# Two gated networks on one TensorE: the low tail weights of gate and value as two 64-row matmuls

## The chip, the cores and the metric

One NeuronCore of one Trainium2 chip. The metric is the device time of one execution in microseconds (us); three runs of the kernel before gave 1295.91, 1297.44 and 1297.57, median 1297.44.

## What is computed

```python
# x: (2, 4096, 192); 8 heads of 24 channels; softmaxed 7-tap causal filter per head
out = np.einsum('hk,bskhg->bshg', w, x_unf)         # token mixing
# first network: 8192 tokens, 192 -> 1536 -> 192
g = x @ w_gate
val = x @ w_val
x = (g * sigmoid(g) * val) @ w_out
# second network: 192 -> 2048 -> 192
h = x @ w_in
y = elu(h) @ w_out2
```

Everything is float32. The change touches the two products `x @ w_gate` and `x @ w_val` alone.

## The kernel before, in words

The 8192 tokens are worked on in 16 chunks of 512, channels on the partitions. TensorE computes with the rounded type fp32r, so each factor is split into a high part (the rounded value) and a low part (what rounding left), and a product is built from several matmuls: high by high, low weights by high data, high weights by low data. The 192 channels are cut into a main part of 128 and a tail of 64. For the tail the 128 rows of the array are filled by keeping the 64 channels twice: `in_b_tail` (in chunk 0 `in_a_tail`) holds the high part of the data in rows 0 to 63 and its low part in rows 64 to 127, and the weights `tail_hi` and `tail_lo` hold the same 64 rows twice. One matmul with `tail_hi` so gives high by high plus high by low, and one with `tail_lo` gives low by high plus low by low. The tile named plain `tail_hi` (not that of a weight) holds the high part of the tail data in both halves; until now only VectorE read it, to make `in_b_tail`.

The hidden layer is worked in blocks of 128 units (f in the first network, 12 of them; k in the second, 16). For a block of the first network TensorE issues ten matmuls of 512 columns: for the gate `main_hi` by high, `main_lo` by high, `main_hi` by low, `tail_hi`, `tail_lo` (`project_up`, which calls `project_main` and `project_tail`, lines 771 to 790), and the same five for the value. The last of each five raises `gate_ready` or `val_ready`. On `gate_ready` ScalarE makes SiLU (line 467), on that and `val_ready` VectorE multiplies (line 634, which raises `mul_done`), ScalarE rounds the product to `hid_hi` (line 480), GpSimd makes `hid_lo` (line 384), and three blocks later TensorE multiplies them with the output weights (`down1`, five matmuls). In the second network a block is five matmuls up and eight shorter ones down (`down2`).

Every engine runs a program of its own, in the order written, and they meet at semaphores. On TensorE it is `mix_phase(0)`, `mix_phase(1)`, a loop of `elu_phase(n)` and `mix_phase(n+1)` for n from 1 to 14, then `elu_phase(15)` and `elu_phase(16)`. A mix phase is the first network of a chunk (with the filter of the next chunk on VectorE), an elu phase the second network of the chunk before. The first block of an elu phase begins with `down1` of block 9 and then waits until the products of all 12 blocks are made, since its bank of PSUM is the value bank of block 11. Gate and value alternate between two banks each. All matmuls pass through the helper `mm`, so all have line 769.

```python
pe.wait_ge(in2_hi, 2 * n)
pe.wait_ge(in2_lo, 2 * n)
if k >= 3:
    pe.wait_ge(elu_done, N2 * (n - 1) + k - 2)
elif last:
    pe.wait_ge(elu_done, N2 * (n - 1) - 2 + k)
elif k == 0:
    pe.wait_ge(mul_done, N1 * (n + 1))
```

Chunk 0 has a piece of its own for its first block, and its phase also takes in the weights as they are loaded; the change leaves chunk 0 as it is.

Of the kernel before, what the change touches and what calls it, by code (L numbers as in the profile page):

```python
# [28 lines left out]
P = 128  # L29


def mix_ffn_ffn(nc, x, weight, w_gate, w_val, w_out1, w_in2, w_out2, out):
# [10 lines left out]
    TAIL = D - P  # L43
# [23 lines left out]
    with ctx:  # L67
        def sb(name, shape, dt=F32):
            return ctx.enter_context(nc.sbuf_tensor(name, shape, dt))

        def sem(name):
            return ctx.enter_context(nc.semaphore(name))


        def split_weight(name, cols):
            return {part: sb(f"{name}_{part}", [P, cols], F32R)
                    for part in ("main_hi", "main_lo", "tail_hi", "tail_lo")}

        gate_w = split_weight("gate_w", F1)
        val_w = split_weight("val_w", F1)  # L80
# [31 lines left out]
        tail_hi = sb("tail_hi", [P, 2, T], F32R)  # L112
# [21 lines left out]
        def input1(c):  # L134
            return in_a if is_int(c, 0) else in_b
# [4 lines left out]
        def is_int(n, value):  # L140
            return isinstance(n, int) and n == value

        def gate_bank(f):
            return up[3] if f % 2 == 0 else up[2]

        def val_bank(f):
            return up[1] if f % 2 == 0 else up[0]
# [24 lines left out]
        gate_ready = sem("gate_ready")  # L172
        val_ready = sem("val_ready")
# [101 lines left out]
        def wait_weights(eng, upto):  # L275

            eng.wait_ge(piece_hi, upto)
            for who, made in (("dve", piece_lo_dve), ("pool", piece_lo_pool)):
                if lo_count(upto, who):
                    eng.wait_ge(made, lo_count(upto, who))  # L280
# [486 lines left out]
        def _(pe):  # L767
            def mm(dst, lhsT, rhs, start, stop):
                return nc.tensor.matmul(dst, lhsT, rhs, start=start, stop=stop, skip_group_check=True)  # L769

            def project_main(bank, w, data, f, lo_ready=None):

                c = slice(f * P, (f + 1) * P)
                mm(bank[:, :], w["main_hi"][:, c], data["hi"][:, :], True, False)
                mm(bank[:, :], w["main_lo"][:, c], data["hi"][:, :], False, False)
                if lo_ready:
                    pe.wait_ge(in1_lo, lo_ready)
                mm(bank[:, :], w["main_hi"][:, c], data["lo"][:, :], False, False)

            def project_tail(bank, w, data, f):  # L780

                c = slice(f * P, (f + 1) * P)
                mm(bank[:, :], w["tail_hi"][:, c], data["tail"][:, :], False, False)
                return mm(bank[:, :], w["tail_lo"][:, c], data["tail"][:, :], False, True)

            def project_up(bank, w, data, f):
                project_main(bank, w, data, f)
                return project_tail(bank, w, data, f)

            def down1(n, f):  # L790


                a, z = f == 0, f == N1 - 1
                hi, lo = hid_hi[:, f % RING, :], hid_lo[:, f % RING, :]
                main_hi, tails = out1_w[:, f, 0:P], out1_w[:, f, P:2 * P]
                main_lo = out1_w[:, f, 2 * P:3 * P]
                if a and is_int(n, 1):
                    pe.wait_ge(y_main_done, 1)
                    pe.wait_ge(halves_done, 1)
                elif a and not is_int(n, 0):  # L800
                    pe.wait_ge(result_done, SUB * (n - 2) + 2)
                if f == 1 and not (is_int(n, 0) or is_int(n, 1)):
                    pe.wait_ge(result_done, SUB * (n - 1))
                pe.wait_ge(hi1_done, N1 * n + f + 1)
                mm(ACC_MAIN[:, :], main_hi, hi, a, False)
                mm(ACC_MAIN[:, :], main_lo, hi, False, False)
                mm(ACC_TAIL[:, :], tails, hi, a, False)
                pe.wait_ge(lo1_done, N1 * n + f + 1)
                mm(ACC_MAIN[:, :], main_hi, lo, False, z)
                mm(ACC_TAIL[:, :], tails, lo, False, z).then_inc(down1_done, 1)  # L810

            def down2(m, k, bank_free=None):


                a, z = k == 0, k == N2 - 1
                pe.wait_ge(hi2_done, N2 * m + k + 1)
                for s in OUT_ORDER if is_int(m, CHUNKS - 1) else range(SUB):
                    if a:
                        bank_free(s)
                    mm(down[s][:, 0:2 * D], hid_hi[:, k % RING, s * P:(s + 1) * P], out2_w[:, k, :], a, False)  # L820
                if is_int(m, CHUNKS - 1) and z:
                    pe.wait_ge(last_lo_done, 1)
                else:
                    pe.wait_ge(lo2_done, N2 * m + k + 1)
                for s in OUT_ORDER:
                    last = mm(down[s][:, 0:D], hid_lo[:, k % RING, s * P:(s + 1) * P], out2_w[:, k, 0:D],
                              False, z)
                    if z:
                        last.then_inc(y_ready, 1)
                if not z:  # L830
                    last.then_inc(down2_done, 1)

            def mix_phase(n):
                chunk0, chunk1 = is_int(n, 0), is_int(n, 1)
                for f in range(N1):
                    if f < LAG:
                        if chunk1:
                            down1(0, N1 - LAG + f)
                        elif not chunk0:
                            down2(n - 2, N2 - LAG + f)  # L840
                    else:
                        if chunk0 and (f - LAG) % OT == 0:
                            wait_weights(pe, (UP_A + 1, OUT_B, PIECES1)[(f - LAG) // OT])
                        down1(n, f - LAG)
                    if chunk0:
                        for g, made in enumerate((UP_A, UP_B, UP_C)):
                            if f * P == GROUPS[g][0]:
                                wait_weights(pe, made)
                    if f == 0 and chunk0:

                        pe.wait_ge(in1_hi, 1)
                        project_main(gate_bank(0), gate_w, in_a, 0, lo_ready=1)
                        project_main(val_bank(0), val_w, in_a, 0)
                        pe.wait_ge(in1_hi, 2)
                        pe.wait_ge(in1_lo, 2)
                        project_tail(gate_bank(0), gate_w, in_a, 0).then_inc(gate_ready, 1)
                        project_tail(val_bank(0), val_w, in_a, 0).then_inc(val_ready, 1)
                        continue
                    if f == 0:
                        pe.wait_ge(in1_hi, 2 * n + 2)  # L860
                        pe.wait_ge(in1_lo, 2 * n + 2)

                    if f >= 2 or chunk1:
                        pe.wait_ge(silu_done, N1 * n + f - 1)
                    elif f == 1 and not chunk0:
                        pe.wait_ge(elu_done, N2 * (n - 2) + N2 - 1)
                    project_up(gate_bank(f), gate_w, input1(n), f).then_inc(gate_ready, 1)
                    if f >= 2 or chunk1:
                        pe.wait_ge(mul_done, N1 * n + f - 1)
                    elif not chunk0:  # L870
                        pe.wait_ge(elu_done, N2 * (n - 2) + N2 - 2 + 2 * f)
                    project_up(val_bank(f), val_w, input1(n), f).then_inc(val_ready, 1)

            def elu_phase(n):
                last = is_int(n, CHUNKS)
# [49 lines left out]
            for k in range(PAIRS):  # L925
                pe.wait_ge(diag_done, k + 1)
                last = mm(MIX0[:, :], diag[:, k, :], paired[:, 2 * k:2 * k + T], k == 0, k == PAIRS - 1)
            last.then_inc(mix0_ready, 1)
            mix_phase(0)
            mix_phase(1)  # L930
            with pe.Fori(1, CHUNKS - 1) as n:
                elu_phase(n)
                mix_phase(n + 1)
# [22 lines left out]
```

## Time and profile before

| | |
|---|---|
| median of three runs | 1297.44 us (1295.91 to 1297.57) |
| profiled execution, span from first to last instruction | 1295.2 us |
| mean granted TensorE clock | 0.998 |
| TensorE matmul busy | 1281.8 us (99%), 6240 matmuls |
| weight loads busy (beside matmuls) | 1084.1 us (84%) |
| VectorE, ScalarE, GpSimd busy | 798.4, 665.3, 656.5 us (62%, 51%, 51%) |
| DMA, mean | 22 GB/s |

The profiled execution lists no time of its own beside its span; the span is 2.2 us under the median of the runs. A matmul's record is longer than the distance to the next one, since matmuls are pipelined: the distance between two starts is what it costs, the record includes the way of the last column to PSUM. Weight loads (PEld) run beside matmuls and have records of their own. A record's start is when the instruction was issued; if its weights are not there yet the record is longer.

### The profile page before, as it was taken

To read this page: it belongs to the slowest core of one execution; us is meant where nothing else is said; L and a number is where in the kernel's file an instruction comes from. 1 tells how busy PE (TensorE), PEld (TensorE's weight loads), DVE (VectorE), ACT (ScalarE), POOL (GpSimd) and SP (SyncE) were. 2 spreads that over 40 slices of the span, in tenths; PEclk is the share of its full clock that TensorE was granted. 3 is DMA by queue.
4 is the path that set the end of the run, shared out by engine and by line. 5 is a ranking of instruction groups with operands and counts; after the bars stand their busy time and mean duration, and the time that the engine had idled before them with its cause. 6 is when DMAs were issued, how large, how long until landed. Compare 5 with 4: busy or idle time off the path is not lost.

```text
span 1295.2 us, 19686 instructions
## 1 busy us (share of the span) xinstructions
PE 1281.8 (99%) x6240; PEld 1084.1 (84%) x6240; DVE 798.4 (62%) x1196; ACT 665.3 (51%) x1104; POOL 656.5 (51%) x477
## 2 busy tenths in 40 slices
PE   7999999999999999999999999999999999999998
PEld 5888888888888888888888888888888888888887
DVE  7667566664665756557565665656666466574675
ACT  5455545455453544545455454554545546355454
POOL 5574445454454544545455454454545545454454
PEclk9999999999999999999999999999999999999999
DMA  8221001010010100101000010100101001010000
GB/s 190 56 75 25 13 9 16 12 24 12 8 21 7 24 12 8 28 0 24 12 14 22 3 21 12 24 12 8 16 12 24 12 8 16 12 24 12 9 13 13
DMA packets 93858, 28.15 MB, mean 22 GB/s; under 512 B 77456, under 2 KB 90256, under 8 KB 93840
## 3 DMA queue, kind: packets, MB, share of 16 engines
q1 hardware_dynamic: 93840, 27.93, 9.6%
q8 instruction: 9, 0.15, 0.1%
q14 instruction: 9, 0.07, 0.0%
HBM read 17.43 MB, written 6.29 MB: 18 GB/s over the span
## 4 chain that ended last, share of the span: by engine, by line
PE 96%; DVE 2%; issue 1%; ACT 0%; POOL 0%; POOLq 0%; DVEq 0%; ACTq 0%
PE up L769 57%; PE down L769 39%; DVE mixed L742 1%; DVE mixed L576 0%; ACT act L498 0%; DVE hidden L634 0%; DVE act L673 0%; DVE hidden L692 0%; DVE out_w L296 0%; ACT out_w L289 0%; DVE in_a_lo L582 0%; POOLq L67 0%; DVE hidden L735 0%; POOL hid_lo L384 0%; POOL head_of L368 0%
## 5 line engine op out<-in xcount | busy, mean ns | idle before, releaser
L384 POOL TENSOR_TENSOR hid_lo<-hidden,hid_hi 128x512 fp32r<-128x512 f32 x447 | 631.0, 1412 | 625.8 <-ACT hid_hi L480 351.0
L634 DVE TENSOR_TENSOR hidden<-act,up 128x512 f32<-128x512 f32 x192 | 131.5, 685 | 275.6 <-ACT act L467 248.5
L519 ACT ACTIVATE hid_hi<-hidden 128x512 fp32r<-128x512 f32 x256 | 162.0, 633 | 209.0 <-DVE hidden L692 209.0
L480 ACT ACTIVATE hid_hi<-hidden 128x512 fp32r<-128x512 f32 x192 | 121.5, 633 | 258.7 <-DVE hidden L634 258.7
L692 DVE SCALAR_TENSOR_TENSOR hidden<-act,up 128x512 f32<-128x512 f32 x256 | 175.9, 687 | 121.8 <-ACT act L498 117.3
L769 PE MATMUL down<-out_w,hid_hi 128*128 128x384 f32 x1024 | 222.9, 339 | 0.4 <-DVE result L619 0.2
L673 DVE TENSOR_SCALAR act<-up 128x512 f32<-128x512 f32 x256 | 176.6, 690 | 63.8 <-PE up L769 58.5
L769 PEld LDWEIGHTS down<-out_w,hid_hi 128*128 128x128 f32 x1024 | 186.7, 188 | 24.2 <-issue 0.6
L498 ACT ACTIVATE act<-act 128x512 f32<-128x512 f32 x256 | 161.3, 630 | 45.7 <-DVE act L673 39.8
L467 ACT ACTIVATE act<-up 128x512 f32<-128x512 f32 x192 | 114.7, 597 | 103.0 <-PE up L769 102.7
L769 PE MATMUL down<-hid_hi,out_w 128*128 128x512 f32 x576 | 166.1, 396 | 0.0
L769 PEld LDWEIGHTS down<-out_w,hid_lo 128*128 128x128 f32 x1024 | 149.2, 189 | 3.8 <-POOL hid_lo L384 3.5
L769 PE MATMUL down<-out_w,hid_lo 128*128 128x192 f32 x1024 | 151.4, 270 | 0.1
L576 DVE SCALAR_TENSOR_TENSOR mixed<-x_t,taps,mixed 128x512 f32<-128x512 f32 x192 | 140.3, 771 | 0.0
L769 PEld LDWEIGHTS down<-hid_hi,out_w 128*128 128x128 f32 x576 | 108.4, 188 | 26.6
L769 PE MATMUL down<-hid_lo,out_w 128*128 128x512 f32 x384 | 121.1, 396 | 0.0
L769 PE MATMUL up<-in_a_hi,in_w_main_hi 128*128 128x512 f32 x240 | 98.7, 411 | 1.6 <-DVE hidden L634 1.6
L769 PE MATMUL up<-in_a_tail,in_w_tail_hi 128*128 128x512 f32 x240 | 95.6, 398 | 0.0
L769 PE MATMUL up<-in_a_lo,in_w_main_hi 128*128 128x512 f32 x240 | 94.7, 395 | 0.0
L769 PE MATMUL up<-in_a_tail,in_w_tail_lo 128*128 128x512 f32 x240 | 94.6, 394 | 0.0
L769 PE MATMUL up<-in_a_hi,in_w_main_lo 128*128 128x512 f32 x240 | 94.5, 394 | 0.0
L769 PEld LDWEIGHTS down<-hid_lo,out_w 128*128 128x128 f32 x384 | 72.3, 188 | 17.6
(141 smaller groups left out, 1772.3 us busy)
## 6 DMA issues: line engine op xcount, KB each, us to landing
x_raw<-x_dram SPq DMA_DIRECT2D x144, 64.0 KB, 2.2
out_dram<-result SPq DMA_DIRECT2D x15, 384.0 KB, 2.6
swapped<-halves SPq DMA_DIRECT2D x32, 128.0 KB, 2.3
stage<-w_out_dram SPq DMA_DIRECT2D x7, 384.0 KB, 3.4
stage<-w_in_dram SPq DMA_DIRECT2D x4, 256.0 KB, 2.9
stage<-w_in_dram SPq DMA_DIRECT2D x8, 128.0 KB, 2.9
stage<-w_gate_dram SPq DMA_DIRECT2D x4, 192.0 KB, 4.0
stage<-w_val_dram SPq DMA_DIRECT2D x4, 192.0 KB, 4.2
```

Source lines behind the costliest of these rows:

```text
L384: return pool.tensor_tensor(hid_lo[:, slot, :], hidden[:, s, :], hid_hi[:, slot, :].bitcast(F32), ALU.subtract)
L467: nc.scalar.activation(act[:, f % 2, :], gate_bank(f)[:, :], ACT.Silu)\
L480: nc.scalar.activation(hid_hi[:, f % RING, :], hidden[:, f % 2, :], ACT.Copy)\
L498: nc.scalar.activation(act[:, k % 2, :], act[:, k % 2, :], ACT.Exp).then_inc(exp_done, 1)
L519: nc.scalar.activation(hid_hi[:, k % RING, :], hidden[:, k % 2, :], ACT.Copy)\
L576: v.scalar_tensor_tensor(mixed[:, part, :], src, tap, mixed[:, part, :], ALU.mult, ALU.add).then_inc(mix_step, 1)
L634: v.tensor_tensor(hidden[:, f % 2, :], act[:, f % 2, :], val_bank(f)[:, :], ALU.mult)\
L673: v.tensor_scalar(act[:, k % 2, :], elu_bank(n, k)[:, :], 0.0, None, ALU.min)\
L692: v.scalar_tensor_tensor(hidden[:, k % 2, :], act[:, k % 2, :], -1.0, elu_bank(n, k)[:, :], ALU.add, ALU.max).then_inc(elu_done, 1)
L742: v.scalar_tensor_tensor(mixed[:, 0, :], src, tap0, mixed[:, 0, :], ALU.mult, ALU.add)\
L769: return nc.tensor.matmul(dst, lhsT, rhs, start=start, stop=stop, skip_group_check=True)
```

## The change

In chunks 1 to 15 the last matmul of the gate and the last of the value are taken out of their places. The value's four others are issued, and then the two low tail products together: the gate's on rows 0 to 63 of the array, the value's on rows 64 to 127, each with 64 rows of weights and of high tail data (`tail_hi[..., 0, :]`). The built program gives both a tile of 64 by 128 of the array, at row 0 and at row 64; all other matmuls of 128 rows have the full tile. The product of low weights by low data is left out. The number of matmuls stays. `gate_ready` is now raised after the value's matmuls too.

```diff
+            def project_most(bank, w, data, f):
+
+                c = slice(f * P, (f + 1) * P)
+                project_main(bank, w, data, f)
+                mm(bank[:, :], w["tail_hi"][:, c], data["tail"][:, :], False, False)
+
+            def project_lo_pair(f):
+
+                c = slice(f * P, (f + 1) * P)
+                top, low = slice(0, TAIL), slice(TAIL, P)
+                mm(gate_bank(f)[:, :], gate_w["tail_lo"][top, c], tail_hi[top, 0, :], False, True)\
+                    .then_inc(gate_ready, 1)
+                mm(val_bank(f)[:, :], val_w["tail_lo"][low, c], tail_hi[low, 0, :], False, True)\
+                    .then_inc(val_ready, 1)
...
-                    project_up(gate_bank(f), gate_w, input1(n), f).then_inc(gate_ready, 1)
+                    if chunk0:
+                        project_up(gate_bank(f), gate_w, input1(n), f).then_inc(gate_ready, 1)
+                    else:
+                        project_most(gate_bank(f), gate_w, input1(n), f)
                     if f >= 2 or chunk1:
                         pe.wait_ge(mul_done, N1 * n + f - 1)
                     elif not chunk0:
                         pe.wait_ge(elu_done, N2 * (n - 2) + N2 - 2 + 2 * f)
-                    project_up(val_bank(f), val_w, input1(n), f).then_inc(val_ready, 1)
+                    if chunk0:
+                        project_up(val_bank(f), val_w, input1(n), f).then_inc(val_ready, 1)
+                    else:
+                        project_most(val_bank(f), val_w, input1(n), f)
+                        project_lo_pair(f)
```

How this moves TensorE's instructions, at an ordinary block of chunk 1. Before:

```order
L769 MATMUL up<-in_b_tail,gate_w_tail_hi 128x512
L769 MATMUL up<-in_b_tail,gate_w_tail_lo 128x512
L769 MATMUL up<-in_b_hi,val_w_main_hi 128x512 [waits mul_done]
L769 MATMUL up<-in_b_hi,val_w_main_lo 128x512
L769 MATMUL up<-in_b_lo,val_w_main_hi 128x512
L769 MATMUL up<-in_b_tail,val_w_tail_hi 128x512
L769 MATMUL up<-in_b_tail,val_w_tail_lo 128x512
L769 MATMUL down<-hid_hi,out_w 128x512 [waits hi1_done]
```

And now, where the shape shown is that of the output:

```order
L769 MATMUL up<-in_b_tail,gate_w_tail_hi 128x512
L769 MATMUL up<-in_b_hi,val_w_main_hi 128x512 [waits mul_done]
L769 MATMUL up<-in_b_hi,val_w_main_lo 128x512
L769 MATMUL up<-in_b_lo,val_w_main_hi 128x512
L769 MATMUL up<-in_b_tail,val_w_tail_hi 128x512
L769 MATMUL up<-tail_hi,gate_w_tail_lo 128x512
L769 MATMUL up<-tail_hi,val_w_tail_lo 128x512
L769 MATMUL down<-hid_hi,out_w 128x512 [waits hi1_done]
```

The gate's last matmul, which completes its bank, moved behind four matmuls of the value; the two with `tail_lo` now stand side by side between full-array ones.

The second place is where the mix phase of chunk 1 ends on TensorE and the first elu phase begins. Now:

```order
L769 MATMUL up<-in_b_tail,val_w_tail_hi 128x512
L769 MATMUL up<-tail_hi,gate_w_tail_lo 128x512
L769 MATMUL up<-tail_hi,val_w_tail_lo 128x512
L953 UNCONDITIONAL_BRANCH
...
L769 MATMUL down<-hid_hi,out_w 128x512 [waits hi1_done]
L769 MATMUL down<-hid_hi,out_w 128x512 x2
L769 MATMUL down<-hid_lo,out_w 128x512 [waits lo1_done]
L769 MATMUL down<-hid_lo,out_w 128x512
...
L769 MATMUL up<-in_a_hi,in_w_main_hi 128x512 [waits mul_done]
```

Between the two low tail matmuls of block 11 and the wait for its product stand five matmuls, as before; but then the gate's bank was complete five matmuls earlier still.

## Rows read from the trace of the kernel before

**Rows 1.** The page: busy time of each engine, granted clock in 40 slices.
```profile
PE 1281.8 (99%) x6240; PEld 1084.1 (84%) x6240; DVE 798.4 (62%) x1196; ACT 665.3 (51%) x1104; POOL 656.5 (51%) x477
...
PE   7999999999999999999999999999999999999998
...
PEclk9999999999999999999999999999999999999999
```
**Rows 2.** The page: the chain that ended last, by engine.
```profile
PE 96%; DVE 2%; issue 1%; ACT 0%; POOL 0%; POOLq 0%; DVEq 0%; ACTq 0%
```
**Rows 3.** Groups of TensorE instructions, the replaced ones: count | busy us, mean ns | idle.
```profile
L769 PE MATMUL up<-in_b_tail,gate_w_tail_lo 128*128 128x512 f32 x180 | 71.5, 397 | 0.0
...
L769 PE MATMUL up<-in_b_tail,val_w_tail_lo 128*128 128x512 f32 x180 | 71.2, 396 | 0.0
```
**Rows 4.** Timeline of TensorE, one block of a mix phase: start us, duration us.
```profile
626.44 0.39 PE L769 MATMUL up<-in_b_hi,gate_w_main_hi 128*128 128x512 f32 x1
...
628.31 0.39 PE L769 MATMUL up<-in_b_tail,val_w_tail_hi 128*128 128x512 f32 x1
628.54 0.40 PE L769 MATMUL up<-in_b_tail,val_w_tail_lo 128*128 128x512 f32 x1
628.78 0.86 PE L769 MATMUL down<-hid_hi,out_w 128*128 128x512 f32 x3
...
629.95 0.39 PE L769 MATMUL up<-in_b_hi,gate_w_main_hi 128*128 128x512 f32 x1
```
**Rows 5.** Timeline of weight loads and matmuls at the start, across a change of rows.
```profile
5.59 0.54 PEld L769 LDWEIGHTS down<-taps_head,head_of 8*128 8x128 f32 x2
5.66 0.57 PE L769 MATMUL down<-taps_head,head_of 8*128 8x7 f32 x2
...
6.15 0.29 PEld L769 LDWEIGHTS up<-fold 128*128 128x128 f32 x1
6.15 0.58 PE L769 MATMUL up<-fold 128*128 128x128 f32 x1
```
**Rows 6.** All matmuls with `fold`: duration min/median/max ns.
```profile
L769 PE MATMUL up<-fold x20: 324/421/582, 4.1 to 9.5; 128*128 128x128 f32 x20
```
**Rows 7.** Timeline of TensorE and its weight loads, where the first elu phase waited.
```profile
102.10 0.19 PEld L769 LDWEIGHTS up<-in_a_hi,in_w_main_hi 128*128 128x128 f32 x1 [2.03 <-DVE hidden L634]
102.10 0.50 PE L769 MATMUL up<-in_a_hi,in_w_main_hi 128*128 128x512 f32 x1 [1.59 <-DVE hidden L634]
102.21 0.19 PEld L769 LDWEIGHTS up<-in_a_hi,in_w_main_lo 128*128 128x128 f32 x1
102.43 0.39 PE L769 MATMUL up<-in_a_hi,in_w_main_lo 128*128 128x512 f32 x1
```
**Rows 8.** Timeline of all engines, the end of a mix phase.
```profile
655.49 0.40 PE L769 MATMUL up<-in_b_tail,gate_w_tail_lo 128*128 128x512 f32 x1
...
655.92 0.60 ACT L467 ACTIVATE act<-up 128x512 f32<-128x512 f32 x1 [0.93 <-PE up L769]
...
656.66 0.40 PE L769 MATMUL up<-in_b_tail,val_w_tail_lo 128*128 128x512 f32 x1
...
657.15 0.69 DVE L634 TENSOR_TENSOR hidden<-act,up 128x512 f32<-128x512 f32 x1 [2.75 <-ACT act L467]
...
657.89 0.19 PEld L769 LDWEIGHTS up<-in_a_hi,in_w_main_hi 128*128 128x128 f32 x1
658.06 0.39 PE L769 MATMUL up<-in_a_hi,in_w_main_hi 128*128 128x512 f32 x1
```
**Rows 9.** Timelines of VectorE and weight loads, the third block of a mix phase.
```profile
623.72 1.15 DVE L619 TENSOR_TENSOR result<-result,down 128x192 f32<-128x192 f32 x4 [0.99 <-ACT result L455]
...
625.03 0.66 PEld L769 LDWEIGHTS down<-hid_hi,out_w 128*128 128x128 f32 x3
```

## The prediction

> **What bounds the kernel now.** I read the page's busy times and granted clock first: TensorE is busy 99% of the span, in every slice but the first, at the full clock of 2.4 GHz (0.998 granted) [rows 1]. The chain that ended last says the same: 96% of it is TensorE [rows 2]. So whatever lengthens or shortens the stream of matmuls moves the time one for one, and other engines count only where TensorE comes to wait for them. Then the groups of matmuls: the two that the change replaces are 180 of the gate and 180 of the value (15 chunks by 12 blocks), with no idle time ahead of them [rows 3]. Their mean of 396 ns is a record, not a cost. The cost is read from the timeline: one block has 15 matmuls of 512 columns and takes 629.95 - 626.44 = 3.51 us, so 0.234 us each [rows 4]. A record of 0.395 us thus has 0.234 us of columns and 0.16 us of way to PSUM.
>
> **The change, part by part.**
>
> *Two full matmuls become two of 64 rows.* If both stream at once, on their two halves of the array, a pair takes 0.234 us where two took 0.469: 180 x 0.234 = 42.1 us less. That is the gross gain, and the whole of it is on the path.
>
> *Full array to halves and back.* The array is cut differently for the pair, so each block gets two changes of cut. The trace before has just one in a stream without a wait: at the start two small matmuls of 8 rows are followed by full-array ones with `fold` [rows 5]. Normally a weight load runs beneath the matmul before it, as the load at 102.21 does, whose matmul starts at 102.43 [rows 7]. Across the change it did not: load and matmul both start at 6.15. The last 8-row record ends at 5.66 + 0.57 = 6.23, its columns were through at 6.23 - 0.16 = 6.07. So the load was held for 0.08 us after the columns were through, and the matmul then waited for its weights: its record is 0.58 us where the median with `fold` is 0.42 [rows 6], 0.16 more. For the fp32r matmuls of this change the price of a load that nothing hides is better read where the first elu phase had waited: 0.50 us against the 0.39 of the next [rows 7], 0.11. I take 0.08 + 0.11 = 0.19 us for a change of cut, and 0.08 + 0.16 = 0.24 as the upper end. The lower end is nothing: it is one event, of fp32 matmuls and an 8-row cut, and it need not hold here. I take the row since it is the only one in which the cut changes. Two changes per block: 0.38 us (0 to 0.48).
>
> The Trainium skill, "TensorEngine Tiling (Array Packing)", Tiling Modes, speaks against this change too: changing the tiling mode, not just the tile, drains TensorE. It has no duration for the drain; the row agrees with it.
>
> *How far the two halves overlap.* The value's half needs its own weights. Behind a change of cut no load was made early, so two loads come one after the other. The nearest distance of two loads with nothing between is 102.21 - 102.10 = 0.11 us [rows 7]. I take 0.11 us by which the value's half starts and ends later; ends are 0 (loads of different rows at once) and 0.234 (one half after the other, no overlap).
>
> By the Trainium skill, "TensorE: Matmul & The Clock Gate", Part 3, matmuls on different row groups start about 4 ns apart; no row of before shows it. By that the skew would be near nothing and the sum 1329 us in place of 1347, the low end of my own case worked out below.
>
> *Per block:* 0.38 + 0.11 - 0.234 = +0.256 us. With 180 blocks: **+46.1 us**. With skew 0: +0.146, 26.3 us. With 0.24 per change and the skew: +0.356, 64.1 us.
>
> *Low by low left out* saves nothing by itself: a matmul of 64 rows streams as many columns.
>
> *The gate's bank is complete later.* Inside a mix phase this has slack: the same bank is asked for two blocks on, and all else on the chain (SiLU, product, rounding, low part) has until three blocks on; the other engines are busy 51 to 62% [rows 1]. There are two tight places. The first is the end of each mix phase. Before, the gate's SiLU started at 655.92, long before the value was ready; the value's last record ended at 656.66 + 0.40 = 657.06, the product started 0.09 later and ended at 657.84, and the elu phase's first weight load started at 657.89, its matmul at 658.06 [rows 8]. Since a load needs 0.11, the matmul could have started at 658.00: 0.06 us of slack. Now SiLU starts only when the pair is through: 0.03 (655.92 after 655.89) + 0.60 + about 0.05 until VectorE sees it puts the product 0.68 us after the pair's end in place of 0.09, so 0.59 later. Were nothing else changed, TensorE would wait 0.59 - 0.06 = 0.53 us. But in my case the gate's half is through 0.11 earlier than the value's, and the five matmuls between start 0.19 later because of the change of cut: 0.53 - 0.11 - 0.19 = 0.23 us, in each of the 15 phases: **+3.5 us**. Queued behind that wait on TensorE is the whole elu phase; nothing catches it up.
>
> The second is the third block, where `down1` needs banks that VectorE reads in the result additions; two of these four must be done, at 623.72 + 1.15/2 = 624.30, and the load stands at 625.03 [rows 9]. ScalarE's copies ahead of them come 0.59 later: 624.89. TensorE comes later too in my case, so this costs nothing. What hides it is 0.14 us of slack; without the changes of cut, `down1` would come 0.234 earlier and wait about 0.1 us, 14 times, 1.4 us.
>
> No DMA, no load and no instruction of the other engines changes, and the granted clock stays at its upper level, since a gap of 2.03 us [rows 7] left no slice with a lower clock [rows 1].
>
> **Sum:** 46.1 + 3.5 = +49.6 us on the median of 1297.4: **1347 us**. The durations are those of the execution with a span of 1295.2 us, 2.2 us under that median; the same distance is kept.
>
> **The rivals.**
>
> *Faster: the change of cut costs nothing.* Loads for 64 rows are made early like any other, because each block has room for two loads (0.11 each) beneath one matmul (0.234). For it: the only evidence against it is one event [rows 5] with another type of matmul. Then -42.1, plus 15 x 0.53 = 8.0 for the ends of the phases and 1.4 for the third blocks: -32.7, 1265 us. If the value's load does wait for the gate's half to start (skew 0.11): 180 x -0.124 = -22.3, plus 15 x 0.42 = 6.3: -16.0, 1281 us. This decides at 0.12 us per change of cut: two of them use up 0.234 us, and above that the pair is slower than the two it replaces.
>
> *The halves don't overlap, and the cut is paid:* 180 x 0.38 = 68.4, plus 15 x (0.53 - 0.23 - 0.19) = 1.6: +70, 1367 us. Against it: two halves of different rows and different banks have nothing to share.
>
> *The change does not do what it says:* the halves are run like full matmuls, one after the other, at no price for the cut. Then nothing is gained per block, and the late gate costs 15 x (0.53 - 0.23) = 4.5 us: 1302 us. A cheap change of cut (0.1 us) with a skew lands beside it, between 1295 and 1310.
>
> **How the numbers follow.** My case, cut paid and halves beside each other, 0.55: from 26.3 + 15 x (0.53 - 0.19) = 31.4, 1329 us, to 64.1 + 15 x (0.53 - 0.11 - 0.24) = 66.8, 1364 us. Faster rival 0.28, in two halves at 1265 and 1281. No overlap 0.07. Near no change 0.10, of which 0.04 within 0.2% (2.6 us, about what a measurement of this kernel can tell from no change) and 0.06 slower. So faster 0.28, same 0.04, slower 0.55 + 0.07 + 0.06 = 0.68. The range takes in the faster rival and goes up to 1362: it leaves out the rival without overlap and the top of my own case, some 0.13 in all. It is wide because the cases of both signs need it; the likeliest one's own range is 1329 to 1364.
>
> **What would show each step.** In the timeline of a block: matmul with `tail_hi` of the value, then a load of 64 rows that starts no sooner than 0.3 us after it (right: cut paid) or beneath it (wrong). The two halves' starts 0.11 us or less apart, by records of 64 rows. The load of the next `down1` 0.3 us after the halves' start, not beside them. A block of 3.77 us in place of 3.51; 3.28 would be the faster rival. At the phase ends, TensorE idle ahead of `in_a_hi,in_w_main_hi`, released by VectorE line 634, some 0.1 to 0.5 us, 15 times. The prediction is wrong if the loads of the halves lie beneath full matmuls, or if the halves start 0.234 us apart.

## The result, and the profile after

| | before | after |
|---|---|---|
| median of three runs | 1297.44 us | 1330.01 us (1327.41 to 1330.26) |
| ratio | | 1.0246, 95% interval 1.0227 to 1.0264 |
| span of the profiled execution | 1295.2 us | 1328.5 us |
| mean granted TensorE clock | 0.998 | 0.997 |

The change makes the kernel slower by 32.6 us, 2.5%; the forecast was 49.6 us slower, 1347 us, in a range that goes from the faster rival up to 1362 us.

The page of the kernel after, busy times and chain by engine. Against [rows 1] and [rows 2] matmul records cover more time and weight loads less (78% for 84%); the chain is TensorE's as before. The clock is at its upper level in all slices but the first, which is looked at below:

```profile
PE 1314.7 (99%) x6240; PEld 1036.9 (78%) x6240; DVE 797.7 (60%) x1196; ACT 667.7 (50%) x1104; POOL 653.8 (49%) x477
...
PEclk8999999999999999999999999999999999999999
...
PE 96%; DVE 2%; issue 1%; ACT 0%; POOL 0%; POOLq 0%; DVEq 0%; ACTq 0%
```

The replaced matmuls of the kernel after, in groups (count | busy us, mean ns | idle before), to be read against [rows 3]: the records went from 397 to 493 ns.

```profile
L769 PE MATMUL up<-tail_hi,gate_w_tail_lo 64*128 64x512 f32 x180 | 88.8, 493 | 0.0
L769 PE MATMUL up<-tail_hi,val_w_tail_lo 64*128 64x512 f32 x180 | 88.7, 493 | 0.0
```

The timeline of TensorE in a block of the kernel after (start us, duration us), which answers to [rows 4]:

```profile
642.99 0.39 PE L769 MATMUL up<-in_b_hi,gate_w_main_hi 128*128 128x512 f32 x1
...
644.63 0.40 PE L769 MATMUL up<-in_b_tail,val_w_tail_hi 128*128 128x512 f32 x1
644.95 0.49 PE L769 MATMUL up<-tail_hi,gate_w_tail_lo 64*128 64x512 f32 x1
644.96 0.49 PE L769 MATMUL up<-tail_hi,val_w_tail_lo 64*128 64x512 f32 x1
645.38 0.97 PE L769 MATMUL down<-hid_hi,out_w 128*128 128x512 f32 x3
...
646.65 0.40 PE L769 MATMUL up<-in_b_hi,gate_w_main_hi 128*128 128x512 f32 x1
```

And its weight loads:

```profile
644.39 0.19 PEld L769 LDWEIGHTS up<-in_b_tail,val_w_tail_hi 128*128 128x128 f32 x1
644.95 0.18 PEld L769 LDWEIGHTS up<-tail_hi,gate_w_tail_lo 64*128 64x128 f32 x1 [0.36 <-issue]
644.95 0.18 PEld L769 LDWEIGHTS up<-tail_hi,val_w_tail_lo 64*128 64x128 f32 x1
645.38 0.53 PEld L769 LDWEIGHTS down<-hid_hi,out_w 128*128 128x128 f32 x3 [0.24 <-issue]
```

A block now takes 646.65 - 642.99 = 3.66 us for 3.51. Into the pair: the value's matmul with `tail_hi` starts at 644.63, its columns are through 0.234 later, at 644.86, the loads of the pair start at 644.95 (0.09 held), and the pair's records are 0.49 for 0.39 (0.10 of waiting for weights). Out of it: the halves' columns are through at 644.95 + 0.10 + 0.23 = 645.28, the next load starts at 645.38 (0.10 held), and the first of the three matmuls of `down1` has its weights 0.11 later (three take 0.97 us for 0.86). Together 0.40; from the block, 3.66 + 0.234 - 3.51 = 0.38 (the sums below use 0.388). Both halves start and end together: their loads start within 0.01 us. By the records the pair's load starts 0.08 us ahead of the end of the matmul before it (644.63 + 0.40 = 645.03), so it isn't held until that matmul has ended; ends of matmuls are modelled in these profiles, so this is less sure than the starts.

The end of a mix phase in the kernel after, all engines, against [rows 8]:

```profile
674.29 0.49 PE L769 MATMUL up<-tail_hi,val_w_tail_lo 64*128 64x512 f32 x1
...
674.82 0.60 ACT L467 ACTIVATE act<-up 128x512 f32<-128x512 f32 x1 [1.68 <-PE up L769]
...
675.45 0.69 DVE L634 TENSOR_TENSOR hidden<-act,up 128x512 f32<-128x512 f32 x1 [2.90 <-ACT act L467]
...
676.19 0.19 PEld L769 LDWEIGHTS up<-in_a_hi,in_w_main_hi 128*128 128x128 f32 x1 [0.47 <-DVE hidden L634]
676.19 0.50 PE L769 MATMUL up<-in_a_hi,in_w_main_hi 128*128 128x512 f32 x1
```

SiLU starts 0.04 us behind the pair (674.82 against 674.78), the product waits for it, ends at 676.14, and the elu phase's first load follows; the matmul waits for its weights besides. From the last pair of matmuls of `down1` (0.63 us, of which 0.47 is cost, from 675.52) TensorE would have gone on at 675.99; it had its weights at 676.19 + 0.10. The loss is 0.3 us per phase.

The first and last start of the value's low tail matmul, by tile, in the kernel before and the kernel after:

```profile
L769 PE MATMUL up<-in_b_tail,val_w_tail_lo x180: 390/397/400, 60.3 to 1212.1; 128*128 128x512 f32 x180
```

```profile
L769 PE MATMUL up<-tail_hi,val_w_tail_lo x180: 491/492/502, 62.1 to 1244.7; 64*128 64x512 f32 x180
```

Between first and last the time grew from 1151.8 to 1182.6 us: 30.8. That is 179 blocks at 0.154 us (0.388 in and out, less 0.234), 27.6, and some 0.3 us at 14 phase ends less what the end of chunk 1, which waits for VectorE anyway, takes back. Of the 33.3 us between the spans 1.8 lie ahead of the first pair, in code that the change doesn't touch. There the clock was at its lower level for longer. Busy times and granted clock (the third figure from the right) from 16 to 24 us, in the kernel before and the kernel after; from there to the first pair the clock is 1.00 in both:

```profile
16.00:24.00 8.00, 7.37 (x25) 5.48 (x26) 7.94 (x12) 5.41 (x9) 3.27 (x3) 0.79 1.14 219
```

```profile
16.00:24.00 8.00, 6.78 (x16) 5.08 (x17) 7.92 (x11) 5.15 (x9) 3.28 (x3) 0.57 1.00 205
```

In both a part of these 8 us was granted at 1.2 GHz, behind a stretch in which TensorE had waited 3 us for the first chunk's data, and the rest at 2.4 GHz. A mean of 0.79 over 8 us costs 0.21 x 8 = 1.7 us of work, one of 0.57 costs 3.4, so the difference is 1.7 of the 1.8 us. The kernel before also has runs between 1295.9 and 1299.0, so a few microseconds in a comparison of two runs can be the clock's; times between two starts later in the trace, such as the 3.66 us, don't have this uncertainty.

### The profile page after: what moved, and what is told of

Its sections match the earlier page's. It is cut to its first block, busy times and chain, and to the rows that moved or that the text cites. A ratio compares the mean times of both kernels' runs of the same rounds, so it can differ in the third digit from the quotient of the medians.

```text
span 1328.5 us, 19686 instructions
## 1 busy us (share of the span) xinstructions
PE 1314.7 (99%) x6240; PEld 1036.9 (78%) x6240; DVE 797.7 (60%) x1196; ACT 667.7 (50%) x1104; POOL 653.8 (49%) x477
## 4 chain that ended last, share of the span: by engine, by line
PE 96%; DVE 2%; issue 1%; ACT 0%; POOL 0%; POOLq 0%; DVEq 0%; ACTq 0%
PE up L769 55%; PE down L769 41%; DVE mixed L742 1%; DVE mixed L576 0%; DVE hidden L634 0%; ACT act L498 0%; DVE act L673 0%; DVE hidden L692 0%; DVE out_w L296 0%; ACT out_w L289 0%; DVE in_a_lo L582 0%; POOLq L67 0%; DVE hidden L735 0%; POOL hid_lo L384 0%; POOL head_of L368 0%
## 5 line engine op out<-in xcount | busy, mean ns | idle before, releaser
L769 PE MATMUL down<-out_w,hid_hi 128*128 128x384 f32 x1024 | 225.8, 342 | 0.3 <-DVE result L619 0.2
L769 PE MATMUL down<-hid_hi,out_w 128*128 128x512 f32 x576 | 182.1, 424 | 0.0
L769 PEld LDWEIGHTS down<-hid_hi,out_w 128*128 128x128 f32 x576 | 96.5, 188 | 48.8 <-issue 32.7
L769 PE MATMUL up<-tail_hi,gate_w_tail_lo 64*128 64x512 f32 x180 | 88.8, 493 | 0.0
```

## The experiments

The theory: every change between the full array and halves of it costs about 0.19 us, half of it a hold of the next load until the columns before are through, half a load that nothing hides; the halves themselves overlap fully; the late gate is a small rest. The rivals: a large part of the loss is the late gate; the price belongs to the two halves beside each other; halves are slow in themselves. The kernel before was run beside each set, with a median of 1297.6 us each time.

### The order of the change without the halves

```diff
-                mm(gate_bank(f)[:, :], gate_w["tail_lo"][top, c], tail_hi[top, 0, :], False, True)\
+                mm(gate_bank(f)[:, :], gate_w["tail_lo"][:, c], in_b["tail"][:, :], False, True)\
                     .then_inc(gate_ready, 1)
-                mm(val_bank(f)[:, :], val_w["tail_lo"][low, c], tail_hi[low, 0, :], False, True)\
+                mm(val_bank(f)[:, :], val_w["tail_lo"][:, c], in_b["tail"][:, :], False, True)\
```

> The order of the changed kernel, but both low tail matmuls on the full array with 128 rows of weights and data, as before the change. Theory 1 (each change of the array's cut costs about 0.19 us, and the late gate costs little): without the cuts 180 x 0.388 us go, two full matmuls cost 0.234 us more per block than the pair; what is left over the kernel before is the late gate alone: 15 phase ends of 0.3 to 0.5 us, +4.5 to +8 us, 1302 to 1306 us. Theory 2 (a good part of the 32.6 us is the late gate, the wait for the product at the phase ends and for the result additions): +15 us or more.

Measured 1303.87 us, ratio to before 1.0043 (1.0029 to 1.0056): +5.6 us (6.2 between the medians). The end of a mix phase, all engines:

```profile
661.50 0.40 PE L769 MATMUL up<-in_b_tail,val_w_tail_lo 128*128 128x512 f32 x1
...
661.70 0.60 ACT L467 ACTIVATE act<-up 128x512 f32<-128x512 f32 x1 [1.53 <-PE up L769]
...
663.08 0.19 PEld L769 LDWEIGHTS up<-in_a_hi,in_w_main_hi 128*128 128x128 f32 x1 [0.44 <-DVE hidden L634]
663.08 0.50 PE L769 MATMUL up<-in_a_hi,in_w_main_hi 128*128 128x512 f32 x1
```

At the phase ends the late gate costs this: the elu matmul starts 1.58 us after the value's last in place of 1.40 [rows 8], and waits 0.1 more for its weights, 0.28 us in 15 phases, 4.2. The blocks themselves take 3.51 us as before. The spans of the profiled runs differ by 7.1 us, and most of the other 2.9 can be put down to the clock: its mean was 0.57 over 16 to 24 us (0.79 before) and 0.89 over 100 to 115 us, behind the wait at the end of chunk 1 (1.00 before), worth 1.7 us each. In this run the gate is ready one matmul, 0.234 us, ahead of the value; in the changed kernel it is not, but there the way out of the cut holds the five matmuls between for 0.19 us, so its loss of 0.3 us is nearly the same. So 4 to 5 of the 32.6 us are the gate's, and the rest is the pair's, but for some 1.7 us of clock.

### Halves apart

Each 64-row matmul alone, in the place that its full matmul had before the change:

```diff
-            def project_up(bank, w, data, f):
+            def project_half(bank, w, data, f, rows):
+                c = slice(f * P, (f + 1) * P)
                 project_main(bank, w, data, f)
-                return project_tail(bank, w, data, f)
+                mm(bank[:, :], w["tail_hi"][:, c], data["tail"][:, :], False, False)
+                return mm(bank[:, :], w["tail_lo"][rows, c], tail_hi[rows, 0, :], False, True)
```

> The kernel before, with each low tail matmul left in its old place but with 64 rows (gate on the upper half, value on the lower); low by low is left out. Theory 1 (the price is paid per change of cut): two pairs of changes per block, each 0.388 us, and no overlap: +180 x 0.776 = +140 us, about 1437 us. Theory 2 (the price belongs to the two halves running side by side, for instance that their loads or reads get in each other's way): the single halves cost little, under +20 us.

Measured 1434.66 us (a single run), +137.0 where the theory had +140. Timeline of TensorE in a block:

```profile
639.06 0.40 PE L769 MATMUL up<-in_b_tail,gate_w_tail_hi 128*128 128x512 f32 x1
639.39 0.50 PE L769 MATMUL up<-tail_hi,gate_w_tail_lo 64*128 64x512 f32 x1
639.82 0.50 PE L769 MATMUL up<-in_b_hi,val_w_main_hi 128*128 128x512 f32 x1
640.16 0.40 PE L769 MATMUL up<-in_b_hi,val_w_main_lo 128*128 128x512 f32 x1
```

From 639.06 to 640.16 three matmuls take 1.10 us instead of 3 x 0.234 = 0.70: 0.40 for one way in and out, around a single half with nothing beside it. So the price does not belong to two halves side by side; it is paid where full-array and 64-row matmuls meet. That it is not one of 64-row matmuls as such is shown by the runs with many of them in a row, below.

### Both on the same half

```diff
-                mm(val_bank(f)[:, :], val_w["tail_lo"][low, c], tail_hi[low, 0, :], False, True)\
+                mm(val_bank(f)[:, :], val_w["tail_lo"][top, c], tail_hi[top, 0, :], False, True)\
```

> The changed kernel with both 64-row matmuls on the upper half of the array (the value's weights and data of rows 0 to 63, which hold the same values). Theory 1 (the halves of the changed kernel overlap in full, which gives 0.234 us per block back): the two now stream one after the other with the second load hidden, +180 x 0.234 = +42 us, about 1372 us. Rival (nothing overlapped in the changed kernel either, the records start together but the columns don't): 1330 us as the changed kernel.

Measured 1366.87 us (a single run), 36.9 more than the changed kernel. Groups:

```profile
L769 PE MATMUL up<-tail_hi,gate_w_tail_lo 64*128 64x512 f32 x180 | 89.7, 498 | 0.0
L769 PE MATMUL up<-tail_hi,val_w_tail_lo 64*128 64x512 f32 x180 | 70.7, 393 | 0.0
```

Only the first of the two waits for weights (498 ns); the second's load was hidden (393). 180 x 0.234 = 42.1 us for streaming one after the other, less 15 x 0.234 = 3.5 for the phase ends, where the gate is now ready 0.234 us ahead of the value: 38.6. The last 1.7 us agree with the clock's share: this run had a mean of 0.79 between 16 and 24 us, as the kernel before, and the kernel after 0.57. So in the changed kernel the halves do overlap in full, and the gross gain of 42 us is there; it is the way in and out, 180 x 0.388 = 70 us, that eats it.

### Halves throughout

If only the change of cut is dear, it should be made rarely. In blocks 3 to 11 of chunks 1 to 15 all matmuls that TensorE issues, up and down, are made of an upper and a lower half (the `down1` of the last three blocks, which stand in the elu phase, stay whole); two halves that stand beside each other write different banks, and a semaphore orders the two halves of one bank. Low by low is left out in these blocks; blocks 0 to 2 and the second network are as before the change. The heart of it:

```diff
+                tops = g_top + m_top + t_top + v_top
+                lows = v_low + t_low + g_low + m_low
+                assert len(tops) == len(lows) == 14
...
+                    if slot == 8:
+                        pe.wait_ge(low_done, 3 * before + 2)
...
+                    i = tops[slot]()
...
+                    i = lows[slot]()
```

(g and v are the halves of gate and value, five on one side and four on the other, since a tail half gives high by high, high by low or low by high; m and t are the three main and two tail halves of `down1`.)

> Chunks 1 to 15, blocks 3 to 11 of the first network: every matmul (up and down) is cut into an upper and a lower half of 64 rows, in 14 slots of two halves on different banks instead of 15 full matmuls; low by low left out there. Blocks 0 to 2 are as before the change. The cut changes twice per phase, not twice per block. Theory 1 (only a change of cut holds up loads, in one cut the loads of halves are hidden like any other): -135 x 0.234 + 30 x 0.19 = -26 us, about 1271 us. Theory 2 (64-row matmuls can't have their loads hidden, or four instructions don't fit in a slot of 0.234 us): at least 0.1 us more in each of 135 x 14 slots, over 1450 us; in between, if the slots take 0.25 us, about 1300 us.

Measured 1286.64 us, ratio 0.9915 (0.9900 to 0.9930): faster than before, but some 16 us short of the estimate. Weight loads in a block:

```profile
641.42 0.18 PEld L771 LDWEIGHTS up<-in_b_hi,gate_w_main_hi 64*128 64x128 f32 x1
641.87 0.18 PEld L771 LDWEIGHTS down<-hid_hi,out_w 64*128 64x128 f32 x1 [0.26 <-PE down L771]
641.87 0.18 PEld L771 LDWEIGHTS up<-in_b_hi,gate_w_main_lo 64*128 64x128 f32 x1
```

A load waits for TensorE itself: the upper half of the tail product asks for the end of the lower half on its bank, a slot too early. It and the load beside it start together at 641.87 and are then not hidden. The waits of the whole run:

```profile
PEld down L771 <- PE down L771: 35.9, 135, 0.3
```

135 times, once per block. No other wait in that list comes once per block.

### The same, with that wait a slot later

```diff
-                tops = g_top + m_top + t_top + v_top
+                tops = g_top + m_top + v_top[:1] + t_top + v_top[1:]
...
                     if slot == 8:
-                        pe.wait_ge(low_done, 3 * before + 2)
+                        pe.wait_ge(low_done, 3 * before + 1)
-                    if slot == 10:
-                        pe.wait_ge(low_done, 3 * before + 1)
+                    if slot == 9:
+                        pe.wait_ge(low_done, 3 * before + 2)
...
-                    if slot in (4, 7, 9):
+                    if slot in (4, 7, 10):
```

> As e4_halves_throughout, but the upper halves of the tail product are moved from slots 8 and 9 to 9 and 10 (an upper half of the value takes slot 8), so that the wait for the lower half on the same bank comes a slot later. In e4 that wait held two loads for 0.27 us once per block, 135 times, and its matmuls' records were 0.49 us in place of 0.39. Theory 1 (14 slots of 0.234 us and two changes of cut per phase are all there is): 1286.6 - 135 x 0.10 = 1273 us, near the 1271 first expected. Theory 2 (the rest comes from streams of halves themselves, slots a little longer than 0.234 us): 1283 to 1287 us.

Measured **1274.97 us, ratio 0.9827 (0.9814 to 0.9841)**: 22.6 us less than the kernel before and 55 less than the change. Weight loads from one block to the next:

```profile
640.20 0.18 PEld L771 LDWEIGHTS up<-in_b_lo,gate_w_main_hi 64*128 64x128 f32 x1
640.21 0.18 PEld L771 LDWEIGHTS up<-in_b_lo,val_w_main_hi 64*128 64x128 f32 x1
640.43 0.19 PEld L771 LDWEIGHTS up<-in_b_tail,gate_w_tail_hi 64*128 64x128 f32 x1
640.44 0.18 PEld L771 LDWEIGHTS up<-in_b_tail,val_w_tail_hi 64*128 64x128 f32 x1
...
643.48 0.18 PEld L771 LDWEIGHTS up<-in_b_lo,gate_w_main_hi 64*128 64x128 f32 x1
```

643.48 - 640.20 = 3.28 us for 14 slots, 0.234 each, with two loads and two matmuls in every slot. The full rate holds in halves as in the full array. The estimate was 1273 us, and from chunk 2 on it comes true: a chunk takes 77.63 us (from 182.10 to 259.73, between the starts of two elu phases) for 79.36 (from 181.96 to 261.32) in the kernel before, 1.73 less, where 9 x 0.234 - 0.38 gives 1.73. Chunk 1 gives nothing. At its end TensorE waits for VectorE in the kernel before already [rows 7], the wait only gets longer (3.4 us for 2.0), and behind it the mean granted clock was 0.89 over 100 to 115 us, where the kernel before has 1.00.

### Two blocks in one stretch of halves

The changed kernel, with the four low tail halves of two blocks issued together in blocks 2 to 9; blocks 0, 1, 10 and 11 are as before the change.

```diff
-                    if chunk0:
+                    if chunk0 or f < 2 or f >= 10:
...
                         project_most(val_bank(f), val_w, input1(n), f)
-                        project_lo_pair(f)
+                        if f % 2 == 1:
+                            project_lo_pair(f - 1)
+                            project_lo_pair(f)
```

> The changed kernel, but in blocks 2 to 9 of each phase the 64-row matmuls of two blocks (four halves, four banks) stand in one stretch of the cut; blocks 0, 1, 10 and 11 are as before the change. Theory 1 (in and out of the cut costs 0.388 us whatever stands between, and a pair of halves saves 0.234 us): per two blocks 0.388 - 0.469 = -0.081 us, 4 x 15 times, -4.9 us, 1292 to 1294 us, just faster than before. Theory 2 (each pair of halves carries a price of its own): slower than before, about 1297 + 60 x 0.31 = 1316 us if nothing is shared.

Measured 1305.32 us, ratio 1.0057 (1.0043 to 1.0071): a miss in the time, though the mechanism is there. Timeline of TensorE:

```profile
641.82 0.40 PE L769 MATMUL up<-in_b_tail,val_w_tail_hi 128*128 128x512 f32 x1
642.15 0.50 PE L769 MATMUL up<-tail_hi,gate_w_tail_lo 64*128 64x512 f32 x1
642.15 0.49 PE L769 MATMUL up<-tail_hi,val_w_tail_lo 64*128 64x512 f32 x1
642.49 0.39 PE L769 MATMUL up<-tail_hi,gate_w_tail_lo 64*128 64x512 f32 x1
642.49 0.39 PE L769 MATMUL up<-tail_hi,val_w_tail_lo 64*128 64x512 f32 x1
```

The second pair pays nothing of its own, and two blocks take about 0.07 us less than before. But the elu phases wait longer at their start. Theory 1 was right about the cut and wrong in taking the rest of the kernel as free.

> As e6_two_blocks_per_cut, with blocks 8 and 9 as before the change too, so that only blocks 2 to 7 share cuts in twos. In e6 two blocks together took 6.96 us against 7.03 (the gain expected), but the phase ends waited 0.54 us more and the first of them 3.1 us more. Theory 1 (the loss of e6 is the backlog of products at the phase end, since both products of a group become ready at once two blocks before it): with two more full blocks behind the last group the backlog is gone, 3 x 15 x -0.07 = -3 us, 1294 us. Theory 2 (the loss belongs to the groups, wherever they stand): still slower than before, 1300 us or more.

The edit is `f >= 8` for `f >= 10`. Measured 1305.85 us, ratio 1.0065 (1.0051 to 1.0078): a miss again, and the loss doesn't go away with two more full blocks behind the last group. VectorE's timeline in a mix phase of this kernel:

```profile
650.82 1.78 DVE L582 TENSOR_TENSOR in_a_lo<-y_main,in_a_hi 128x512 fp32r<-128x512 f32 x1
652.53 0.67 DVE L634 TENSOR_TENSOR hidden<-act,up 128x512 f32<-128x512 f32 x1
653.12 1.40 DVE L576 SCALAR_TENSOR_TENSOR mixed<-x_t,taps,mixed 128x512 f32<-128x512 f32 x2
654.45 1.77 DVE L585 SCALAR_TENSOR_TENSOR in_a_tail<-tail_hi,lo_half,y_tail 128x512 fp32r<-128x512 f32 x1
656.15 0.67 DVE L634 TENSOR_TENSOR hidden<-act,up 128x512 f32<-128x512 f32 x1
...
658.67 2.89 DVE L576 SCALAR_TENSOR_TENSOR mixed<-x_t,taps,mixed 128x512 f32<-128x512 f32 x2
661.48 0.67 DVE L634 TENSOR_TENSOR hidden<-act,up 128x512 f32<-128x512 f32 x1
...
663.34 0.69 DVE L634 TENSOR_TENSOR hidden<-act,up 128x512 f32<-128x512 f32 x1 [1.10 <-ACT act L467]
```

In the blocks that also prepare the second network's input, VectorE has 656.15 - 652.53 = 3.62 us of work for a block of 3.51 us: no slack at all. That is so in the kernel before too, where two such products also start 3.62 us apart, and there VectorE catches up in the block behind. Here it doesn't. It works without an idle stretch from 650.82 to 662.24, and two steps of the filter that take 1.40 us elsewhere take 2.89 from 658.67 on. GpSimd's and ScalarE's rows beside them:

```profile
657.57 1.74 POOL L384 TENSOR_TENSOR hid_lo<-hidden,hid_hi 128x512 fp32r<-128x512 f32 x1 [1.89 <-ACT hid_hi L480]
659.49 1.52 POOL L384 TENSOR_TENSOR hid_lo<-hidden,hid_hi 128x512 fp32r<-128x512 f32 x1 [0.18 <-ACT hid_hi L480]
...
662.19 0.63 ACT L480 ACTIVATE hid_hi<-hidden 128x512 fp32r<-128x512 f32 x1 [2.29 <-DVE hidden L634]
662.73 0.58 ACT L467 ACTIVATE act<-up 128x512 f32<-128x512 f32 x1
```

VectorE is behind: the product that starts at 658.07 has had its value bank complete since 655.29 + 0.39 = 655.68. It follows that of 656.15 closely, so GpSimd's two low parts come 0.18 us apart, from 657.57 to 661.01, and the slow filter steps lie beside them. In this trace and in that of the run before, 28 filter steps behind 140 us, two in each of 14 chunks, take 1.2 or 1.8 us in place of 0.74, always in this place, 20.7 us more in all; in all other kernels of this document none does there. The product behind them comes at 661.48, ScalarE, which works in order, can round it only at 662.19, and makes the last SiLU only at 662.73, though its gate was complete at 661.55. So the last product, which the elu phase waits for, is late. VectorE itself stands idle for 1.10 us just ahead of it.

Not all of the loss is there. The spans are 9.0 and 7.8 us longer than that of the kernel before, and 6.0 and 4.6 of these are there by the start of chunk 2 (at 145.85 and 144.44 us, against 139.85): the end of chunk 1 waits 5.1 us for VectorE in place of 2.0, and the mean granted clock behind it is 0.77 and 0.89 over 100 to 115 us, for 1.00. The 14 chunks behind lose 0.2 us each, which is 0.5 at the phase end less what the groups gain. That VectorE, 62% busy on the average, is full just there, and slower beside two low parts in a row, was read from the traces; no run with less work on VectorE or GpSimd was made to show it.

## Why the prediction was right

- **The stream of matmuls sets the time.** Held from chunk 2 on in every run but the last two: the times of a chunk follow from counts of 0.234 us slots, changes of cut and the phase end. In the last two VectorE makes the phase end longer.
- **The gross gain of 42.1 us** is real (37 us come back when the halves share a side, with 3.5 for the phase ends and 1.7 for the clock taken off).
- **The price of a change of cut**, taken from one event at the start of the trace of before [rows 5] and a load that nothing hid [rows 7]: 0.08 + 0.11 = 0.19, twice per block 0.38. Measured 0.38 to 0.40: 0.09 and 0.10 held, 0.10 and 0.11 of waiting for weights. That two rows of other kinds of matmul add up so closely is in part luck; the prediction itself gave 0 to 0.48. The rule of the Trainium skill ("TensorEngine Tiling (Array Packing)", Tiling Modes) that a change of mode drains TensorE agrees with the trace, which shows the next load held for 0.09 to 0.10 us.
- **The skew between the halves, taken as 0.11 us, was the term that was mis-sized.** It is under 0.01 us. The loads of the two halves start together; the distance of 0.11 us in [rows 7] is that of two loads for the same rows, and doesn't hold for different ones. 180 x 0.11 = 19.8 us too much, against a miss of 17.0 in all; the other way went about 1 us at the phase ends and 1.7 us of clock, which no term of the sum had. The estimate given beside the Trainium skill's Part 3 of "TensorE: Matmul & The Clock Gate", 1329 us, was the right one: its rule of nearly equal starts agrees with this trace (644.95 and 644.96).
- **The phase ends**: 0.23 us forecast, about 0.3 measured, since the gate's half is not ahead of the value's (0.53 - 0.19 = 0.34 by the prediction's own terms). 4 to 5 us, not 3.5.
- **The third blocks, nothing:** held. From the start of the third block to that of the fourth, across this `down1`, it is 3.68 us for 3.53 in the kernel before, 0.15 more, as in every other block. The wait that was forecast for the case without a price for the cut was not put to the test.
- **The granted clock** was taken as unchanged. It is from 24 us on; ahead of that its mean was 0.57 for 0.79 in the profiled runs, worth about 1.7 us.

The faster rival (no price for the cut) and the one without overlap are both excluded, by the block of 3.66 us and by the two matmuls on the same half, and so is the case in which the halves are run like full matmuls, whose block would be 3.51 us.

## What to carry to other kernels

Matmuls of 64 rows side by side give all that they promise, a pair for the time of one, but going from full-array matmuls to halves and back costs 0.19 us each way, in the midst of a dense stream, where a full matmul of 512 columns costs 0.234. One pair per stretch of halves loses 0.15 us. Two gain 0.07 us per stretch on TensorE, which here was more than lost again on VectorE. Nine blocks of a phase in halves gain all that was counted, from chunk 2 on (1297.6 to 1275.0 us here). So before a matmul is packed, count the changes of cut, not the matmuls. And where a product is made available later, look at each engine in that stretch rather than at its average: VectorE at 62% had blocks with no slack.

## What the runs showed of the hardware that was not expected

- The loads for two different halves start within 0.01 us of each other, also when neither was made early (644.95 both); loads for the same rows are 0.11 us apart [rows 7].
- In a stretch of halves each slot of 0.234 us takes two loads and two matmuls, and 14 slots take 3.28 us: no loss against the full array.
- A wait of TensorE on its own earlier matmul costs a load that isn't hidden, about 0.1 us, when only one slot lies between; with two no such wait is left in the trace. A chunk with nine such blocks took 78.46 us in the first run and 77.63 in the second, 0.09 per block.
- Steps of the filter on VectorE take 1.2 and 1.8 us in place of 0.74 where two low parts on GpSimd follow each other 0.18 us apart.
- The same kernel's time moves by a few microseconds with the clock granted to TensorE: the kernel after took 1330.26 us in a run with a mean of 0.997 and 1327.41 in one with 1.000.
